# Sparse attention with a two-expert MoE on one core: each expert tile adds its weighted rows into the output in DRAM, in place of a combine stage at the end

## The reference, cut to what matters

```python
# attention: 4 batches x 8 heads, 576 tokens, 64 features, only the 32 highest scores of a row are kept
x = attention(q, k, v) as (N, D) = (2304, 512)
noisy_logits = x @ w_gate + log1p(exp(x @ w_noise)) * noise          # (N, 8)
top2 = np.argpartition(-noisy_logits, 2, axis=1)[:, :2]              # two experts of a token
top2_w = softmax of the two logits                                   # their weights
out = np.zeros((N, D), dtype=np.float32)
for e in range(E):                                                   # 8 experts
    for k in range(2):
        mask = top2[:, k] == e
        h = np.maximum(x[mask] @ w1[e], 0.0)                         # w1[e] is 512 x 1024
        out[mask] += top2_w[mask, k, None] * (h @ w2[e])             # w2[e] is 1024 x 512
```

## Time and profile before

| what | value |
|---|---|
| median of 3 runs | 1536.6 us (1531.18 to 1542.96) |
| the profiled execution | 1543.03 us |
| its span, first to last instruction | 1540.9 us |
| mean granted PE clock, share of full speed | 0.802 |
| PE busy | 1304.4 us (85%) |
| DVE busy | 917.8 us (60%) |
| POOL busy | 599.6 us (39%) |
| ACT busy | 584.0 us (38%) |

### The profile page before, as it was taken

The page is one execution under the profiler, slowest core; times in us unless marked ns, Lnnn a source line. Parts: engine busy times, 40 slices in busy tenths (PEclk is TensorE's granted clock), DMA queues, the critical chain, the costliest instruction groups (busy, mean ns, idle before and its releaser), DMA issues. The chain is left out here.

```text
span 1540.9 us, 20197 instructions
## 1 busy us (share of the span) xinstructions
PE 1304.4 (85%) x5768; PEld 1004.9 (65%) x5769; DVE 917.8 (60%) x1770; ACT 584.0 (38%) x1181; POOL 599.6 (39%) x428
## 2 busy tenths in 40 slices
PE   6899998889988899888957449999999999999940
PEld 3666666666665666656647347877878787788830
DVE  6999889999899998999920443133131322311112
ACT  2544444544444444444412114334242442422222
POOL 3654556656556555665530022032030212210036
PEclk9956667876778767787555559999999999999975
DMA  5001000110001100100021015141341314111038
GB/s 160 25 25 32 16 24 24 31 31 15 24 24 31 31 20 19 30 26 16 9 65 66 1 64 209 41 144 65 127 147 41 143 41 150 41 41 47 28 106 282
DMA packets 79468, 94.84 MB, mean 62 GB/s; under 512 B 47888, under 2 KB 47888, under 8 KB 79440
## 3 DMA queue, kind: packets, MB, share of 16 engines
q1 hardware_dynamic: 66928, 62.51, 12.7%
q0 software_dynamic: 6320, 20.71, 4.4%
q10 hardware_dynamic: 6192, 11.27, 1.9%
HBM read 73.77 MB, written 20.71 MB: 61 GB/s over the span
## 5 line engine op out<-in xcount | busy, mean ns | idle before, releaser
L315 POOL TENSOR_SCALAR probs<-scores,top 128x576 f32<-128x576 f32 x144 | 249.4, 1732 | 323.1 <-ACT expd L339 264.7
L585 PEld LDWEIGHTS ps_o<-vA,pT 128*128 128x128 f32 (+3 forms) x1600 | 272.8, 240 | 115.3 <-issue 66.2
L585 PE MATMUL ps_o<-vA,pT 128*128 128x128 f32 (+3 forms) x1600 | 336.5, 365 | 4.2 <-ACT pT L354 4.2
L410 DVE MAX8 top<-work 128x8 f32<-128x576 f32 x432 | 304.7, 747 | 0.0
L677 POOL COPY tile_rows<-table 128x1 uint32 (+1 forms) x43 | 36.1, 839 | 515.7 <-PE ps_x L823 397.0
L552 PE MATMUL ps_s<-kT,qT 64*128 64x288 f32 x512 | 219.1, 563 | 9.4 <-DMA q_mid<-q_t 6.9
L404 DVE MATCH_REPLACE8 work<-top,work 128x576 f32<-128x576 f32 x288 | 211.7, 743 | 0.0
L319 POOL TENSOR_TENSOR probs<-probs,expd 128x576 f32<-128x576 f32 x144 | 202.7, 1408 | 12.0
L570 PE MATMUL ps_p<-ident,probs 128*128 128x128 f32 x576 | 124.2, 352 | 76.7 <-POOL probs L319 76.2
L795 DVE TENSOR_TENSOR hl<-ps_s,hh 128x512 fp32r<-128x512 f32 x86 | 55.3, 685 | 224.2 <-ACT hh L732 224.2
L840 PE MATMUL ps_h<-w1h,xh 128*128 x344 | 140.7, 409 | 30.4 <-DVE xl L782 30.4
(11 more groups left out here) (124 smaller groups left out, 1657.8 us busy)
## 6 DMA issues: line engine op xcount, KB each, us to landing
raw<-w SPq DMA_DIRECT2D x16, 2048.0 KB
ys_dram<-y_sb ACTq DMA_DIRECT2D x43, 256.0 KB, 2.0
qT<-q_t SPq DMA_DIRECT2D x16, 288.0 KB, 2.8
kT<-k_t SPq DMA_DIRECT2D x16, 288.0 KB, 2.9
xt<-x_dram SPq DMA_DIRECT2D x2, 2304.0 KB, 12.0
out<-raw SPq DMA_DIRECT2D x18, 256.0 KB
vA<-v SPq DMA_DIRECT2D x32, 128.0 KB, 2.2
x_dram<-o_fin SPq DMA_DIRECT2D x32, 128.0 KB, 2.0
```

The source lines that it names most:

```text
L315: nc.gpsimd.tensor_scalar(probs[:, s % PRING, :], scores[:, s % RING, :], top[:, s % RING, ROUNDS - 1, 7:8], None, ALU.is_ge).then_inc(mas ...
L410: nc.vector.max(top[:, r, n + 1, :], work[:, a, :])\
L585: mm = nc.tensor.matmul(ps_o[a:z, 0:VW], pT[0:rows, s % 2, c * P + a:c * P + z], vA[u][0:rows, h, c, :], start=(c == 0), stop=(c == KB))
```

## The change

ys_dram and the combine stage go. x_dram has one row more, row N, of zeros. At the start, `out` and that row are filled with zeros by 19 DMAs on SP's queue, behind the loads of the first two pairs and ahead of the router's loads; POOL makes the zeros (128x512) ahead of its other constants. The table matmul has 86 columns in place of 43: 43 for the row number (kept as N minus the token, so that a padding slot comes out as row N) and 43 for the weight of the slot, which is read into `slot_weight`. The weights are therefore computed ahead of the table matmul.

In the second block, ACT loses the copy of ps_y and its DMA. DVE gets a scalar_tensor_tensor at the end of step n: y_sb = ps_y * slot_weight[n] + prev. `prev` holds the rows of `out` that tile n's tokens have so far; POOL gathers them and scatters the sum back. Rows with number N are left out by the bounds check of both DMAs. POOL's gather of x keeps its text, but is now called from `step` with the others.

```diff
-    x_dram = nc.dram_tensor("x_dram", (N, D), F32, kind="Internal").ap()
-    ys_dram = nc.dram_tensor("ys_dram", (MAXT * P, D), F32, kind="Internal").ap()
+    x_dram = nc.dram_tensor("x_dram", (N + 1, D), F32, kind="Internal").ap()
...
+            sp.wait_ge(zeros_ready, 1)
+            sp.dma_start(x_dram[N:N + 1, :], zeros[0:1, :]).then_inc(zero_out, 16)
+            for t in range(T):
+                sp.dma_start(out[t * P:(t + 1) * P, :], zeros[:, :]).then_inc(zero_out, 16)
...
+            nc.gpsimd.memset(zeros[:, :], 0.0).then_inc(zeros_ready, 1)
...
-            nc.gpsimd.iota(token[:, :], [[P, T]], base=0, channel_multiplier=1,
+            nc.gpsimd.iota(token[:, :], [[-P, T]], base=N, channel_multiplier=-1,
...
             for c in range(2):
-                half = tile_hot[:, c * T:(c + 1) * T, :]
-                link(nc.vector.tensor_tensor(half, iota_p..., part_f..., ALU.is_equal))
-                link(nc.vector.tensor_tensor(half, half, token..., ALU.mult))
+                at_row = tile_hot[:, c * T:(c + 1) * T, 0:MAXT]
+                at_weight = tile_hot[:, c * T:(c + 1) * T, MAXT:2 * MAXT]
+                link(nc.vector.tensor_tensor(at_weight, iota_p..., part_f..., ALU.is_equal))
+                link(nc.vector.tensor_tensor(at_row, at_weight, token..., ALU.mult))
+                link(nc.vector.tensor_tensor(at_weight, at_weight, weight..., ALU.mult))
...
-            link(nc.vector.tensor_copy(table[:, :], ps_h[:, 1, 2 * T * E:2 * T * E + MAXT]))
+            link(nc.vector.tensor_scalar(table[:, :], ps_h[:, 1, 2 * T * E:2 * T * E + MAXT], -1.0, float(N), ALU.mult, ALU.add))
+            link(nc.vector.tensor_copy(slot_weight[:, :], ps_h[:, 1, 2 * T * E + MAXT:2 * T * E + 2 * MAXT]))
...
-                mm = nc.tensor.matmul(ps_h[:, 1, 2 * T * E:2 * T * E + MAXT], lane_hot[:, n, :], tile_hot[:, n, :],
+                mm = nc.tensor.matmul(ps_h[:, 1, 2 * T * E:2 * T * E + 2 * MAXT], lane_hot[:, n, :], tile_hot[:, n, :],
...
 POOL, second block
+            def gather_prev(n, u):
+                if not (isinstance(n, int) and n == 0):
+                    pool.wait_ge(scattered, 16 * n)
+                pool.sem_inc(outs_ready, -1)
+                nc.gpsimd.tensor_copy(out_rows[:, u:u + 1], table[:, bass.ds(n, 1)]).then_inc(outs_ready, 1)
+                pool.wait_ge(outs_ready, 1)
+                nc.gpsimd.indirect_dma_start(
+                    out=prev[:, u, :], out_offset=None, in_=out,
+                    in_offset=bass.IndirectOffsetOnAxis(ap=out_rows[:, u:u + 1], axis=0),
+                    bounds_check=last_row, oob_is_err=False).then_inc(prev_in[u], 16)
+            def scatter(n, u):
+                pool.wait_ge(y_ready, n + 1)
+                pool.sem_inc(tiles_out, 1)
+                nc.gpsimd.indirect_dma_start(
+                    out=out, out_offset=bass.IndirectOffsetOnAxis(ap=out_rows[:, u:u + 1], axis=0), in_=y_sb[:, u, :],
+                    in_offset=None, bounds_check=last_row, oob_is_err=False).then_inc(scattered, 16)
             gather(0, 0)
             gather(1, 1)
-            with pool.Fori(1, MAXT // 2) as m:
-                for u in range(2):
-                    gather(2 * m + u, u)
-            gather(MAXT - 1, (MAXT - 1) % 2)
-            pool.wait_ge(ys_written, 1)
-            (36 gathers of the combine stage)
+            nc.gpsimd.memset(prev[:, :, :], 0.0).then_inc(prev_clear, 1)
+            pool.wait_ge(prev_clear, 1)
+            pool.wait_ge(zero_out, 16 * (T + 1))
+            gather_prev(0, 0)
+            def step(n, u):
+                if exists(n, 2):
+                    gather(n + 2, u)
+                scatter(n, u)
+                if exists(n, 1):
+                    gather_prev(n + 1, 1 - u)
+            steps(pool, step)
+            pool.wait_ge(scattered, 16 * MAXT)
...
 ACT, second block
-                act.wait_ge(y_done, n + 1)
-                nc.scalar.activation(y_sb[:, u, :], ps_y[:, :], ACT.Copy).then_inc(y_copied, 1)
-                act.dma_start(ys_dram[bass.ds(n * P, P), :], y_sb[:, u, :]).then_inc(y_out[u], 16)
...
 DVE, second block, end of step
+                dve.wait_ge(y_done, n + 1)
+                dve.wait_ge(prev_in[u], 16 * ((n - u) // 2) + 16)
+                nc.vector.scalar_tensor_tensor(out=y_sb[:, u, :], in0=ps_y[:, :], scalar=slot_weight[:, bass.ds(n, 1)],
+                                               in1=prev[:, u, :], op0=ALU.mult, op1=ALU.add).then_inc(y_ready, 1)
...
 PE, results_of
-                    pe.wait_ge(y_copied, n)
+                    pe.wait_ge(y_ready, n)
```

More of the change, by code:

```diff
@@ L82, in sparse_attention_moe_kernel @@
         table = sb("table", [P, MAXT], U32)
+        slot_weight = sb("slot_weight", [P, MAXT])
         tile_rows = sb("tile_rows", [P, 2], U32)
-        slot = sb("slot", [P, 2, T], I32)
-        weight = sb("weight", [P, 2, T])
+        out_rows = sb("out_rows", [P, 2], U32)
         raw1 = sb("raw1", [P, DC, F])
@@ L93, in sparse_attention_moe_kernel @@
         scope = phase
+        zeros = sb("zeros", [P, D])
+        slot = sb("slot", [P, 2, T], I32)
+        weight = sb("weight", [P, 2, T])
         ones = sb("ones", [P, P])
@@ L151, in sparse_attention_moe_kernel @@
         const_step = sem("const_step")
+        zeros_ready = sem("zeros_ready")
+        zero_out = sem("zero_out")
         ones_ready = sem("ones_ready")
@@ L200, in sparse_attention_moe_kernel @@
         y_done = sem("y_done")
[L201 to L207, removed]
+        y_ready = sem("y_ready")
+        outs_ready = sem("outs_ready")
+        tiles_out = sem("tiles_out")
+        prev_clear = sem("prev_clear")
+        prev_in = [sem(f"prev_in{u}") for u in range(2)]
+        scattered = sem("scattered")
         block = phase.enter_context(nc.Block())
@@ L531, in _ @@
             link(nc.vector.reciprocal(weight[:, 0, :], weight[:, 1, :]))
-            nc.vector.tensor_tensor(weight[:, 1, :], gap[:, :], weight[:, 0, :], ALU.mult).then_inc(weights_ready, 1)
+            link(nc.vector.tensor_tensor(weight[:, 1, :], gap[:, :], weight[:, 0, :], ALU.mult))
+            for c in range(2):
+                at_row = tile_hot[:, c * T:(c + 1) * T, 0:MAXT]
+                at_weight = tile_hot[:, c * T:(c + 1) * T, MAXT:2 * MAXT]
+                link(nc.vector.tensor_tensor(at_weight, iota_p[:, 0:MAXT].unsqueeze(1).to_broadcast([P, T, MAXT]),
+                                             part_f[:, 1, c, :].unsqueeze(2).to_broadcast([P, T, MAXT]), ALU.is_equal))
+                link(nc.vector.tensor_tensor(at_row, at_weight, token[:, :].unsqueeze(2).to_broadcast([P, T, MAXT]), ALU.mult))
+                link(nc.vector.tensor_tensor(at_weight, at_weight, weight[:, c, :].unsqueeze(2).to_broadcast([P, T, MAXT]), ALU.mult))
+            nc.vector.memset(picked[:, 0, 0:1], 0.0).then_inc(hot_ready, 1)
+            dve.wait_ge(table_done, 1)
+            link(nc.vector.tensor_scalar(table[:, :], ps_h[:, 1, 2 * T * E:2 * T * E + MAXT], -1.0, float(N), ALU.mult, ALU.add))
+            link(nc.vector.tensor_copy(slot_weight[:, :], ps_h[:, 1, 2 * T * E + MAXT:2 * T * E + 2 * MAXT]))
+            nc.vector.memset(picked[:, 0, 0:1], 0.0).then_inc(slots_ready, 1)
         @block.tensor
@@ L633, in sparse_attention_moe_kernel @@
         y_sb = sb("y_sb", [P, 2, D])
-        pick = [raw1[:, :, :].rearrange("p c f -> p (c f)"), raw2[:, :, :].rearrange("p c f -> p (c f)")]
+        prev = sb("prev", [P, 2, D])
         ps_t, ps_y = ps_s, ps_o
         FH = FC // 2
-        RINGO = 8
         block = ctx.enter_context(nc.Block())
@@ L660, in _ @@
                 sp.dma_start(raw2[:, :, :], w2[bass.ds(e, 1), :, :].rearrange("a (c p) n -> p (a c) n", p=P)).then_inc(w_in, 16)
[L661 to L666, removed]
         @block.gpsimd
@@ L745, in step @@
                     hi_x(n + 2)
-                act.wait_ge(y_done, n + 1)
-                if not (isinstance(n, int) and n < 2):
-                    act.wait_ge(y_out[u], 16 * ((n - u) // 2))
-                nc.scalar.activation(y_sb[:, u, :], ps_y[:, :], ACT.Copy).then_inc(y_copied, 1)
-                act.wait_ge(y_copied, n + 1)
-                act.dma_start(ys_dram[bass.ds(n * P, P), :], y_sb[:, u, :]).then_inc(y_out[u], 16)
-            steps(act, step)
[L755 to L764, removed]
+            steps(act, step)
         @block.vector
```

25 lines of the change are left out of this document (4 added, 21 removed).

## The result

The changed kernel takes 1796.78 us (median of 4, 1787.85 to 1803.66) against 1539.78 before: a ratio of 1.1668, 95% interval 1.1582 to 1.1753. Forecast were 1732 (1650 to 1800) with a chance of 0.94 for slower: right in sign and cause, with two terms too small, and only 3 us inside the upper end of the range. The time is that of rival A (1797), and so is its mechanism, to which I had given 0.16. A ratio leaves out executions over 1.5% above the shortest of their kernel, a median does not, so the two need not agree to the last digit.

The account below looks back on a forecast made before the run. PE bounds the tiles; POOL's in-order queue would make it wait for x. Ordinary tiles 172, openings 60, step 1 10, routing 5, start 0, end -52: +195 us, 1732 us on the median, range 1650 to 1800.

Parts of the forecast that it names:

- rival A: Tile stage: same stall, clock at 1.2 GHz behind every gap, openings blocked behind both weight operations; +260, 1797 us; chance 0.16.
- The loop: Ordinary tiles: x gather queued on POOL behind scatter and gather_prev; loop 16.49 us against PE's 12.28, PE waits 4.2.
- The clock: PE's gap per tile: granted clock falls six times in ten at 1.67 us, 1.0 us per tile, bounds 0 and 2.2.
- The openings: Six steps where an expert's weights are prepared: POOL collides with DVE; 26.5 us per step, +60, bounds +6 and +86.
- the first of three outcomes: At an opening, POOL's x gather gets its row numbers between DVE's two weight operations; 26.5 us for the step.
- What is taken off ACT: 0: ACT loses its copy and DMA issue in the tiles; ACT is no bound, so 0 us.
- Routing: Two more DVE operations, one small copy and 86 table columns on the path: +4.8 us, bounds 2 and 8.
- Step 1: Step after tile 0: late DVE operation, then scatter and gathers beside a weight load; about 25 us, +10, bounds 0 and 18.
- The end: After the last y, the 56.9 us combine goes and 4.8 us are left: -52 us.
- The zeros at the start: Start: 19 DMAs and 4.7 MB of zeros, ahead of loads needed long after; 0 us, bounds 0 and 12.

Follow-up runs that it names:

- x_one_ahead: Changed kernel with POOL issuing the gather of x for tile n+3, not n+2, at the head of step n: 1491.25 us, ratio 0.9759.
- no_landing_wait: Changed kernel with the scatter going to a tensor of its own, so the gather of prev need not wait for its landing: 1600.79 us, ratio 1.0431.
- no_prev: Changed kernel without the gather of the rows so far; POOL still waits for the scatter's landing and copies row numbers: 1696.75 us, ratio 1.1049.
- pe_kept_busy: Changed kernel with 16 more matmuls of 512 columns on PE ahead of its wait for x: 1737.85 us, ratio 1.1276.
- low_parts_tiny: Changed kernel with DVE's low parts of the next expert's weights cut to 8 columns at openings: 1744.05 us, ratio 1.1424.
- no_weight_traffic: Changed kernel with the raw weight loads of experts 1 to 7 cut to 32 KB in place of 2 MB: 1762.75 us, ratio 1.1462.
- busy_tiny_no_traffic: Changed kernel with low parts cut to 8 columns, raw weights of experts 1 to 7 to 32 KB, and 16 more matmuls on PE: 1654.19 us, ratio 1.0772.

## Why the prediction was right, and where it was too low

**The loop.** Right, and the reason for the sign. The sum of rows gave 10.23 us from add to turn of x; 10.15 were measured. That it fits so closely is in part luck, since two of its terms were off and cancelled: POOL's start behind DVE is 0.87, not 0.50, and from the scatter's start to the next copy are 2.93 us, not 3.3 + 0.25. x_one_ahead shows that the order alone makes the stall, no_landing_wait that it is a sum of terms; no_prev shortens it too, but by 0.7 us less than its sum said.

**The clock.** The mis-sized term. I took a fall behind six gaps in ten at 1.67 us, 1.0 per tile. It was a fall at every gap, 3.4 or 6.9 us long in the two windows shown. Over the 33 ordinary tiles the time from the turn of x to the next add has a mean of 8.56 us in place of 6.26, so a fall cost 2.3 us per tile, 33 x 1.3 = 43 us above the forecast; the loop up to the turn has a mean of 10.3, another 3 us. pe_kept_busy gives 2.0 us per tile back. "Three of six" came from gaps of 2.9 and 3.6 us, some 60 us and more apart, and I raised it only to six in ten for 4.2. In no_landing_wait, where a shorter gap comes in every tile, 16 of 33 had a fall, and in no_prev, at gaps of 2.6 to 3.7 us in every tile, all 34. So a gap like those of the kernel before was followed by a fall far more often once it came in every tile; why was not tried. The rule that I set beside it (the Trainium skill, TensorE: Matmul & The Clock Gate, section on HAM oscillation: every tile begins cold) describes what the trace of the changed kernel shows: in all 40 steps the turn of x took 1.07 to 1.12 us in place of 0.60.

**The openings.** I took +60 us and the first of three outcomes, 26.5 us per step; it was the second, behind both operations, 31.1 (forecast 30.9): +82.5. That 30.9 came so close has luck in it too: POOL is free 15.0 us after the loop's start, not 16.5, and the rows land 7.8 us behind that (1255.40 to 1263.23), where I took 5.9. The step that failed is "What is taken off ACT: 0". It is true for ordinary tiles. But without its copy and DMA issue ACT begins hh and then w1h 1.5 us sooner after the loop's start, 1241.89 - 1240.40 = 1.49 against 1130.33 - 1127.36 = 2.97, and so w1l begins at 5.37 where I had 6.85. POOL's copy comes at 6.16: in my sum it was just ahead of w1l, in the trace behind it. I had seen that this was decided on an edge and had left one of its two sides at its old place. no_landing_wait shows the other side of the edge. That ACT's earlier start is what moved w1l is read from these starts; no kernel here delays it again. That DVE's two operations and not ACT's work or the weight loads make most of an opening's length is shown by low_parts_tiny and no_weight_traffic.

**The rest.** Routing +2.4 for +4.8: the 72 PE records with 86 columns take 15.66 us from first to last, those with 43 took 15.59, a median of 421 ns each against 420. So their columns do not set their length: of the 2.6 us that I had for them, 0.1 was measured. Step 1 +8.4 for +10, tile 0 +2.6 (part of it DVE's add standing behind xl and the low parts, which I had counted in step 1). The end -51.0 for -52. The zeros at the start: SP issues its first load behind them at 48.51 us in place of 47.72 and the first rows of x at 86.44 in place of 84.53, the next at 137.41 in place of 137.78; a cost beyond that would be lost in the spread of the attention phase (below). The errors by themselves: +46 in the ordinary tiles, +22.5 at the openings and -2 in the small ones, together the 66 us between the forecast of +195 and the 260.9 between the two profiled spans. One reading in the forecast was off: losses of 247 us against a gain of 52 are a gain paid 4.7 times over, not "almost four times".

## What to carry to other kernels

An in-order queue passes on its longest wait to everything behind it: before adding a dependent transfer, list what comes next on that engine and when its reader wants it; if that is needed earlier, issue it earlier, which here turned 17% slower into 2.5% faster. When work is moved off an engine that "is no bound", recompute when its next operations start, since they may meet something new. And a stall of a few microseconds per tile is to be priced with the clock that PE has after it, here more than half of the stall itself once again. How often it falls cannot be taken over from a kernel in which such stalls are rare.

## What the runs showed of the hardware that I had not expected

- The end of DVE's add reached POOL's scatter 0.86 to 0.87 us later in the tiles looked at, where a copy's completion on POOL itself reached the next DMA in 0.50.
- An indirect scatter of 128 rows of 2 KB landed faster than the gather: a median of 2.8 us from its start against 3.4.
- A copy of one column on POOL took 3.69 us and the issue of a DMA 4.89 beside DVE operations of two SBUF inputs, where they take 0.18 and 0.99 in an ordinary tile. The copy ended at 1250.25, 0.06 us behind the end of w1l; the DMA's issue, begun at 1250.51, ended at 1255.40, 0.87 us behind the end of w2l, which had begun at 1250.11. So each of the two POOL instructions was caught once.
- The attention phase, whose code is the same in all the kernels from the changed one on, did not end at the same time in the profiled executions: its logits were ready between 828.7 us (low_parts_tiny) and 870.6 (busy_tiny_no_traffic), at mean granted clocks of 0.70 to 0.76 up to there. Stages of two kernels can be compared within the profile; totals only with their intervals.
